# An attention and two MoE layers on one core: the second MoE's w1 sums and splits made by GpSimd during the attention and kept in DRAM

## What is computed

```python
for t in range(S):                       # attention, per batch and head
    y[t] = r[t] @ (state + outer(u * k[t], v[t]))
    state = w[t][:, None] * state + outer(k[t], v[t])
x = (((x @ w1) * (x @ w2)) @ w3) @ w_out # first MoE, d_ff 1024
logits = x @ w_gate; logits -= logits.max()
P = exp(logits)                          # then 8 rounds of row and column scaling
for e in range(8):                       # second MoE, w1[e] 384 x 1024, w2[e] 1024 x 384
    out += P[:, e:e+1] * (maximum(x @ w1[e], 0) @ w2[e])
```

## Time and profile before

| | |
|---|---|
| runs, median (lowest to highest) | 2086.49 us (2085.49 to 2087.83) |
| profiled execution | 2086.09 us, span 2084.3 us, granted TensorE clock 0.992 |
| TensorE busy | 2014.5 us, 97% of the span |
| VectorE, ScalarE, GpSimd busy | 1207.6, 860.1 and 604.3 us (58, 41 and 29%) |
| DMA | 273.61 MB, mean 131 GB/s |

### The profile page before, as it was taken

One profiled execution on the slowest core, in us unless ns is written; L12 is line 12 of the kernel. 1 busy time (PEld: TensorE's weight loads), 2 busy tenths in 40 slices (PEclk: granted clock), 3 DMA queues, 4 the chain that ended last, 5 costly groups with the idle time before them and its releaser, 6 DMA issues.

```text
span 2084.3 us, 39849 instructions
## 1 busy us (share of the span) xinstructions
PE 2014.5 (97%) x16048; PEld 1683.9 (81%) x16048; DVE 1207.6 (58%) x1879; ACT 860.1 (41%) x1577; POOL 604.3 (29%) x661
## 2 busy tenths in 40 slices
PE   6999999999998999999989999999999999999998
PEld 4699999999776778777768888888887888888887
DVE  3666666664686766667664554554465554455454
ACT  4555655554443444444433333333333333333332
POOL 2112112112556776667640111110142110111111
PEclk9999999999999999999989999999999999999999
DMA  8311211200343655555424444434343445343432
GB/s 204 76 47 44 50 46 41 54 17 15 111 171 148 223 192 174 201 196 196 178 108 163 139 163 152 142 139 164 139 152 117 151 139 172 140 158 133 162 132 100
DMA packets 94838, 273.61 MB, mean 131 GB/s; under 512 B 10240, under 2 KB 49088, under 8 KB 86592
## 3 DMA queue, kind: packets, MB, share of 16 engines
q1 hardware_dynamic: 93968, 270.59, 39.3%
q10 hardware_dynamic: 688, 0.48, 0.1%
HBM read 198.58 MB, written 71.27 MB: 129 GB/s over the span
## 4 chain that ended last, share of the span: by engine, by line
PE 61%; issue 24%; POOL 8%; DVE 5%; DMA 1%; ACT 1%; SPq 0%; POOLq 0%; DVEq 0%; ACTq 0%
PE ps L1498 13%; PE ps L1500 13%; PE ps L1499 12%; PE ps L1302 6%; PE ps L1303 5%; PE ps L1304 5%; POOL x L640 3%; PE ps L1375 3%; PE ps L1325 2%; POOL late_sum L637 1%; PE ps L1414 1%; DVE xs_lo L1052 1%; PE ps L1416 1%; DVE h_lo L1235 1%; POOL x L726 1%
## 5 line engine op out<-in xcount | busy, mean ns | idle before, releaser
L1500 PE MATMUL ps<-h_hi,w 128*128 128x512 f32 x1152 | 455.8, 396 | 0.0
L1498 PE MATMUL ps<-h_hi,w 128*128 128x512 f32 x1152 | 454.9, 395 | 0.0
L1499 PE MATMUL ps<-h_lo,w 128*128 128x512 f32 x1152 | 451.3, 392 | 0.0
L988 ACT ACTIVATE h_hi<-tb 128x512 fp32r<-128x512 f32 x378 | 238.7, 633 | 450.0 <-DVE tb L1230 240.1
L773 ACT ACTIVATE tb<-ps 128x512 f32<-128x512 f32 x378 | 226.8, 600 | 461.8 <-PE ps L1500 460.4
L640 POOL TENSOR_TENSOR x<-x,tmp 128x512 f32<-128x512 f32 x126 | 172.2, 1385 | 725.9 <-DVE tmp L1248 724.9
L1226 DVE TENSOR_TENSOR tb<-tb,ps 128x512 f32<-128x512 f32 x252 | 172.0, 685 | 274.7 <-PE ps L1500 264.6
L1235 DVE SCALAR_TENSOR_TENSOR h_lo<-tb,h_hi 128x512 fp32r<-128x512 f32 x378 | 298.2, 790 | 41.9 <-ACT h_hi L988 35.6
L1230 DVE TENSOR_TENSOR tb<-ps,tb 128x512 f32<-128x512 f32 x252 | 173.5, 689 | 215.3 <-PE ps L1500 214.3
L1499 PEld LDWEIGHTS ps<-h_lo,w 128*128 128x128 f32 x1152 | 220.6, 191 | 50.0
L1498 PEld LDWEIGHTS ps<-h_hi,w 128*128 128x128 f32 x1152 | 217.3, 189 | 46.9
(11 more groups left out here) (161 smaller groups left out, 3120.8 us busy)
## 6 DMA issues: line engine op xcount, KB each, us to landing
w<-w_rows SPq DMA_DIRECT2D x128, 384.0 KB, 3.9
early<-early_rows SPq DMA_DIRECT2D x42, 1024.0 KB, 4.8
late<-late_rows SPq DMA_DIRECT2D x42, 896.0 KB, 4.6
w_rows<-w SPq DMA_DIRECT2D x64, 384.0 KB, 6.1
early_rows<-early SPq DMA_DIRECT2D x21, 1024.0 KB, 6.0
late_rows<-late SPq DMA_DIRECT2D x21, 896.0 KB, 4.7
w_raw<-w SPq DMA_DIRECT2D x32, 576.0 KB, 5.8
Pb<-p_rows SPq DMA_DIRECT2D x24, 512.0 KB, 5.9
```

The lines of the kernel that those rows point to most:

```text
L988: nc.scalar.activation(h_hi[:, slot_of(G, b), :], tb[:, t_of(G, b), :], ACT.Relu).then_inc(h_hi_made, 1)
L1498: mm(o, w_hi, x_hi, start=start, stop=False, skip_group_check=True)
L1499: mm(o, w_hi, x_lo, start=False, stop=False, skip_group_check=True)
L1500: return mm(o, w_lo, x_hi, start=False, stop=stop, skip_group_check=True)
```

## The change

The 21 sets of sums and parts of w1 (one for a group of three slices) are no longer made in the groups that use them. A set is made as five batches of three operands, 105 in all, by GpSimd alone: it also makes the high parts. The order of the operands (`MADE`) is such that each batch uses few raw blocks. 66 batches are made in units 1 to 11 of the attention, six a unit, ahead of GpSimd's other work of the unit; 39 in groups 1 to 8 of pass 0, five a group. A batch lies in one of two buffers and SyncE stores it to w1_rows (`keep_batch`); the next batch for this buffer waits for that store. There is one buffer w1_raw; its next load (`load_w1`) follows the store of a set's last batch. All passes, pass 0 too, load `early` and `late` from w1_rows. ScalarE's `take_early` and `take_late` go. To make room ruk shares its place with Ktok (with one more wait of VectorE), the first w2 lies at xw, and `staged` at the place of the batches (with a wait in pass 1).

```diff
-    EARLY = {Q1: 0, S4: 1, R1: 2, S2: 3, Q5: 4, S1: 5, S3: 6, Q0: 7}
-    LATE = {R4: 0, S7: 1, R2: 2, R3: 3, S5: 4, S6: 5, S8: 6}
+    MADE = [Q1, S4, R1, S2, Q5, S1, S3, Q0, R4, S7, R2, S5, S6, R3, S8]
+    BATCH, EARLY = 3, 8
+    BATCHES = NP // BATCH
+    PER_UNIT = 6
...
+        LAST_BATCH = BATCHES * (NG - 1)
+        BEFORE = PER_UNIT * (U - 1)
+        in_unit = lambda u: range(PER_UNIT * (u - 1), PER_UNIT * u)
+        in_group = lambda G: range(min(LAST_BATCH, BEFORE + BATCHES * (G - 1)), min(LAST_BATCH, BEFORE + BATCHES * G))
...
+            def load_w1(n):
+                if n:
+                    sp.wait_ge(w1_made, BATCHES * n)
+                for i, j, e, f in pieces(full_at(n)):
+                    sp.dma_start(w1_raw[:, KD * i:KD * j, :]..., w12[e, :, f:f + j - i, 0:D]).then_inc(w1_loaded, 16)
+
+            def keep_batch(x):
+                n, j = divmod(x, BATCHES)
+                sp.wait_ge(w1_made, x + 1)
+                sp.dma_start(w1_rows[n, :, :, BATCH * j:BATCH * j + BATCH, :], batch[x % 2]...).then_inc(w1_kept[x % 2], 16)
+                if j == BATCHES - 1 and n + 1 < NG - 1:
+                    load_w1(n + 1)
...
             for u in range(1, U + 1):
+                made = in_unit(u) if u < U else ()
...
                     load_r(u + 1)
+                for x in made[0:2]:
+                    keep_batch(x)
...
                     load_w(u + 1)
+                for x in made[2:4]:
+                    keep_batch(x)
...
                     load_v(u + 1)
                 sp.wait_ge(y_copied, 2 * u)
                 move_gap(u - 1)
+                for x in made[4:]:
+                    keep_batch(x)
...
             for G in range(NST * NG):
...
-                if st and g:
+                if g and n:
                     load_late(n)
...
+                made = in_group(G) if g else ()
+                for x in made[0:2]:
+                    keep_batch(x)
+                for i in range(size(G)):
+                    if st == 0:
+                        if i == 2:
+                            load_early(n + 1)
+                            for x in made[2:]:
+                                keep_batch(x)
                         keep_w2(slice_no(G) + i)
...
+                if st == 0 and 0 < g < NG - 1:
+                    load_w2(G + 1)
...
             for u in range(U + 1):
+                if 1 <= u < U:
+                    for x in in_unit(u):
+                        make_batch(x)
                 if u + 1 < U:
                     begin_rpad(u + 1)
...
                 if G == P_TURN[0] + 1:
                     for n in range(6):
                         add_y(n)
+                for x in made[0:2]:
+                    make_batch(x)
                 if g == NG - 1 and st + 1 < NST:
                     sum_xw(st + 1)
                     for p in x_summed_in(st + 1):
                         sum_x(st + 1, p)
-                if st == 0 and g + 1 < NG:
-                    sum_early(G + 1)
-                    add_ys(S3, R2)
-                    split_early(G + 1)
-                    add_ys(R2, NP)
+                add_ys(S3, R2)
+                for x in made[2:]:
+                    make_batch(x)
+                add_ys(R2, NP)
```

More of the change, by code:

```diff
@@ L145, in build_program @@
         xT = sb("xT", [P, KD, CT])
+        made_at = top[0]
+        w1_raw = sb("w1_raw", [P, 9, P])
+        batch_at = [top[0] + i * size_of([P, 2, BATCH, P]) for i in range(2)]
+        batch = [sb(f"batch{i}", [P, 2, BATCH, P], f32r) for i in range(2)]
+        batch_sum = [sb(f"batch_sum{i}", [P, BATCH, P], at=batch_at[i] + size_of([P, BATCH, P])) for i in range(2)]
+        uv = sb("uv", [P, 2, P])
+        assert top[0] <= nc.sbuf_usable_end
         wout_raw = sb("wout_raw", [P, NF, D], at=x2_at)
@@ L193, in build_program @@
         first_raw = sbs("first_raw", [P, KD, P])
-        w1_raw += [sbs("w1_raw1", [P, 9, P])]
-        staged = sbs("staged", [P, 2, D])
+        late = sbs("late", [P, 2, NP - EARLY, P], f32r)
         end_of(W_lo_at)
@@ L245, in build_program @@
             sem, ["w_loaded", "u_loaded", "consts_loaded", "left_loaded", "wout_loaded", "wg_loaded", "first_loaded", "p_stored", "p_loaded"])
-        w1_loaded = [sem(f"w1_loaded{i}") for i in range(2)]
         w2_loaded = [sem(f"w2_loaded{i}") for i in range(2)]
@@ L271, in build_program @@
                   "turned_copied", "stored"])
-        early_kept, late_kept, early_loaded, late_loaded = map(sem, ["early_kept", "late_kept", "early_loaded", "late_loaded"])
+        early_loaded, late_loaded = map(sem, ["early_loaded", "late_loaded"])
+        w1_kept = [sem(f"w1_kept{i}") for i in range(2)]
         w2_kept, w2_again = ([sem(f"{n}{i}") for i in range(W2_RING)] for n in ("w2_kept", "w2_again"))
@@ L521, in _ @@
             sp.wait_ge(up_done, NF * (U - 1))
[L522 removed]
+            load_early(0)
             sp.wait_ge(wg_set, 1)
@@ L527, in _ @@
             sp.wait_ge(down_done, SLICES)
+            sp.wait_ge(xs_split, NP)
             load_w2(0)
+            load_late(0)
             load_w2(1)
-            load_w1(1)
-            keep_early(0)
             for G in range(NST * NG):
@@ L745, in _ @@
                     continue
-                if st == 0 and g > 1:
-                    sum_late(G)
-                    split_late(G)
+                made = in_group(G)
                 ys = [n for p in range(NP) for n in ys_after((G, p)) if n >= 6]
@@ L1041, in _ @@
                         act.wait_ge(stored, 16 * (j - 1))
+                    else:
+                        act.wait_ge(w1_made, LAST_BATCH)
+                        for i in range(2):
+                            act.wait_ge(w1_kept[i], 16 * ((LAST_BATCH + 1 - i) // 2))
                     copy(staged[:, j % 2, :], R_ps[:, 0:D]).then_inc(turned_copied, 1)
```

228 lines of the change are left out of this document (98 added, 130 removed).

## The result

The kernel before takes 2085.99 us in the same session (median; 2084.13 to 2087.83), the changed one 2151.28 us (2145.05 to 2152.35): ratio 1.031, 95% interval 1.029 to 1.033. I had said 2100 us with a range up to 2134. The sign was right, the size was not. The profiled execution took 2151.62 us, its span is 2149.8.

The account below looks back on a forecast made before the run. TensorE, busy 2014.5 of 2084.3 us, was taken as the bound, with gains only where it is below its pace. 2086 - 20 (groups 9 to 20, change of pass) + 7 (attention) + 27 (groups 1 to 8) = 2100 us, range 2070 to 2134.

Parts of the forecast that it names:

- groups 9 to 20: First pass, 748 to 1029 us: waits for sums and parts of w1 go, 12 of 13.5 us gained.
- the change of pass: Group 21 and first to second pass: GpSimd's sum of x no longer waits for split_late, 8 us gained.
- The attention, +7: Attention: 66 batches on GpSimd cost 7 us, 5 for stalls and 2 for late casts; bounds 0 and 25.
- The port: Attention: VectorE slowed by sharing SBUF access with GpSimd, 0.5 us of stall a unit, 5 us in all.
- Rival 2: Attention: VectorE and GpSimd fully exclude each other, units take 46 us instead of 38.9, total 2163; chance 0.07.
- 2 us for the late casts: Attention: GpSimd's cast of x slips behind the sixth batch, with about 4 us of play; 2 us in all.
- Groups 1 to 8, +27: First pass: the chain of batches, stores and loads on GpSimd and SyncE delays TensorE by 27 us; bounds 10 to 50.
- Cycles: Groups 1 to 8: the chain from one group's fifth batch to the next's, taken as 25.5 us; the group wants 22.7.
- extras: Additions to the chain in groups 4, 5 and 6: about 5, 9.3 and 5 us, 19.3 together.
- W: Groups 1 to 8: landing time of the w1 load that the fifth batch needs, taken as 4.8 us.
- Rival 1: Groups 1 to 8: the chain keeps up, these groups between -8 and +2 us, total 2064 to 2076; chance 0.16.
- Passes 1 and 2, 0 forecast: The second and third passes: they read the same bytes as before, so no change.

Follow-up runs that it names:

- e3: e2 with GpSimd waiting in the attention for no store and no load but the first, and the later w1 loads there left out; 2115.09 us.
- e2: The changed kernel with its first load of w1 issued right behind the first load of V, ahead of the last start-up loads; 2142.41 us.
- e6: e2 with GpSimd itself issuing the attention's batch stores and w1 loads on its own DMA queue, in place of SyncE; 2144.27 us.
- e4: The changed kernel with the next group's w2 load issued ahead of the fifth batch's store in groups 1 to 7; 2128.37 us.
- e5: The changed kernel with pass 0's 39 batches spread two a group over groups 1 to 20; 2134.82 us.
- e8: The changed kernel with the first w1 load early, five batches a unit, then three a group, the third's store behind the next w2 load; 2108.52 us.
- e9: e8 with the load of the next group's early part ahead of the stores of the group's first two batches in pass 0; 2085.87 us.
- e7: e4 with the early and late parts kept in two DRAM tensors of their own; 2134.93 us.

## Why the prediction was right or wrong

**The bound and the stretches.** Right: what could be won was won in groups 9 to 20 and at the change of pass. Groups 9 to 20 gave 7.6 us for the 12 taken: a group now takes 22.98 us, and 23.5 to 24.6 in groups 11, 14 and 19, where I had used 22.7 from the second pass, and so all of its "next to nothing" was still to pay. The change of pass gave 8.4 us for 8, and pass 1 began 1.6 us quicker to its first early tile.

**The attention, +7: the step that failed, by 32 us in the profiled run and by 25 to 27 in the three others with this attention.** Two of its estimates held. The port was priced at 5 us and e3 shows 4.1 for all of the work. Rival 2, the price if every overlap reached TensorE, is refuted: the time came near to its 2163 for another reason. Its sign, "a unit of the attention takes over 41 us", even appeared (41.1 to 45.0 us in six of nine units), so that sign can't tell it from late waits; e3 could. VectorE grew by 40 us in 380 and TensorE's pace stayed (e3). Of the instructions that I had named, R and K took longer in the changed kernel (on average 0.95 and 0.97 us, before 0.79 and 0.72; 120 to 500 us), ab_lo did not (0.54, before 0.59). The Trainium skill, SBUF — State Buffer, section "Who interferes with whom", describes that block. VectorE's 237.8 us growing to 277.5 for the same work beside 262 us of GpSimd is of that kind (e3); the rule says nothing of whether somebody waits for VectorE. What failed is "2 us for the late casts", which measured 28 to 35, in three places.
First, unit 1: I did not look where the first w1 load stands in SyncE's queue at the start, though the stretch before 60 us was there to read. It landed 20 us after its issue, and cost 4 to 6 us (e2).
Second, the slack. I had six batches ending 4 to 6 us behind the start of the Rpad copies, and 4 us of play for the cast. That is a calculation that ends within 2 us of the edge in ten units out of ten, and I gave it the value on the good side. GpSimd's own time for six batches was as taken: 263.67 - 54.58 = 209 us in 9.3 units, 22.5 a unit. But the loads of w1 did not take 4 us: where one fell between two batches it held GpSimd for 5.7 to 10.7. The larger part is the load itself, 4.4 to 8.5 us from issue to GpSimd's start; the late issue, behind SyncE's own waits, adds 0.6 to 5.9, median 0.8. Stores held GpSimd for another 40.7 in all, and there the late issue weighs more (e6).
Third, where GpSimd's round is longer than TensorE's, every unit pays the difference; the play of 4 us is used up once. The periods between Rpad copies became 39.4 to 45.0 us instead of 38.9.
The upper bound of 25 us for this term stands without a sum. One for the waits was missing. (A slip beside it: the terms given for five batches alone add up to 16.7 us, not 15.7.)

**Groups 1 to 8, +27: mechanism right, 11 us too small, inside its bounds of 10 to 50.** Most of the signs that I had named are there: TensorE's waits for tb at R1 (groups 2, 5, 6, 7 and 8), load_w2 issued behind the fifth batch (781.77, 12 us into the group that needs it), GpSimd idle for stores and for w1. Waits for late at S5 were not: one, of 0.6 us. Cycles outside the groups with extras took 26.4 to 27.5 us, where I took 25.5: from the issue of w1's load to GpSimd's start it was 4.4 to 5.1 us where I took W = 4.8, and GpSimd's waits for stores were longer. The sum also had its start wrong: group 9 began at 752.26 in the kernel before, not at 749.76, so that its own terms give 24 us and the miss is 14. The extra of group 4 was 9 us, not 5: the third batch stood 14 us for a store that SyncE held behind the stores of P. Group 5 lost 4 instead of 9.3, group 6 7 instead of 5. e4 proves the link: the load of w2 taken out of the chain gave 17.5 of the 38.4 us back. But it was not the only chain. The load of the early part behind the first two stores, which I had not priced, is the next in line and as dear (e5, e8, e9: 23 to 28 us). Rival 1 needed groups near 23 us and is refuted by groups of 25.6 to 34.1; its own terms give 2058 to 2072, not 2064 to 2076.

**Passes 1 and 2, 0 forecast, +1.5 and +2.8.** A small drift without waits: groups 1 to 20 of pass 1 take 23.20 us on average instead of 23.06, those that took 22.74 now 22.98. e7 excludes the layout in DRAM. Its cause is not settled. A step of 1.5 us between executions (499.4 or 500.9, 514.3 or 515.8) is part of what these parts show.

**The count.** In the profiled runs 31.8 us of the miss lie in the attention, 15.4 in pass 0, 4.3 in the two other passes. The chances: I gave 0.93 to outcomes with the attention under 25 us, on a term whose own calculation ended at the edge. That the total came within 12 us of rival 2's is chance.

## What to carry to other kernels

Work that is moved to an engine with idle time costs little while its turn fits that time, waits included, and then it costs in every round: in ten units three or four batches cost about 1 us, five 4.5, six 22 to 28. So when a sum of moved work comes out within a tenth of the slack, price the other side of the edge, and look for the number of pieces just below it. A queue that issues in order makes any load wait for whatever its neighbours wait for; where a load moves behind a store, ask what that store waits for, and ask again after each reordering, since the same reordering gave 27 us with three batches and cost 28 with five.

## What the runs showed that I had not expected

VectorE's instructions can be stretched by a sixth over 380 us (237.8 to 277.5 us busy for 474 and 473 instructions) with TensorE at 99.6% throughout. A DMA issue on GpSimd's own queue takes 0.68 us there, with 0.3 us before it, and one of SyncE's takes about 0.5 us of an engine that has nothing else to do. And a w1 load issued at 48.26 us behind the start-up loads landed after 20 us, where the median for such loads over the whole program was 4.8. Executions of one and the same attention differed by 7 us (576.9 and 583.9), so a single profile is no measure of a change of that size.
